# Writing the attention output of a recurrent-attention and two-layer feed-forward kernel as two column tiles of 64 tokens

## The chip, the cores and the metric

The kernel runs on one core of a Trainium2 chip. The metric is the time of the device for one execution, in microseconds (us), lower is better. Before the change it is 1050.95 us, the median of three runs (1050.66 to 1052.82).

## What is computed

For 4 batches of 8 heads, 768 tokens and a head dimension of 48, a decaying state is carried over the tokens, and its output goes through two feed-forward layers. The core of the reference is:

```python
for t in range(S):
    cur = einsum('bhd,bhe->bhde', u * k[t], v[t])
    y[t] = einsum('bhd,bhde->bhe', r[t], state + cur)
    state = w[t][..., None] * state + einsum('bhd,bhe->bhde', k[t], v[t])
x = y                    # 3072 tokens x 384
h = x @ w_in             # 384 x 2048
g = where(h >= 1, h, where(h <= -1, 0, (h + 1)**2 / 4))
x2 = g @ w_out           # 2048 x 384
out = (silu(x2 @ w_gate) * (x2 @ w_val)) @ w_out2    # 384 x 1536, 1536 x 384
```

## The kernel before, in words

The 3072 tokens are cut into 8 halves of 384 tokens (NG = 8, T = 384; two halves make one sequence), and each half into 3 windows of 128 tokens (NW = 3, WIN = 128). Inside a window the recurrence is written as matrix products: products of r and k inside the window (scores), masked, times the values, plus r times the state carried into the window.

Phase 1 runs the first feed-forward layer of half g in 16 slots (J1 = 16) and puts the attention of half g + 1 into its slots 3 to 12. In a slot TensorE (the engine that the profile calls PE) does `tile_in` (9 products on line 1039), then the slot's one or two attention pieces (`do_fill`, in the order of FILLS), then `tile_out` (9 products on line 1063). The feed-forward products are in fp32r and stream 384 columns each. The attention of half 0 has no feed-forward work to lie beside and runs at the start of the kernel. Phase 2 (from about 600 us on) runs the second feed-forward layer and has no attention in it.

The attention pieces of a window are these, with the lines of their products. All are fp32, and each product written in the code is two matmul records in the trace (a weight load and a matmul for either of two passes), except for transposes:
- KT, line 1082: k transposed, 4 transposes.
- AT, line 1089: the scores. Each of the 8 products has 48 rows of contraction, at partitions 0 to 47 for one head of a pair and 64 to 111 for the other, so the two heads lie on different halves of the array's rows. They write two banks. This is the only code of the kernel in which products occupy different parts of the array.
- ST, line 1098: the state's increment, 4 products with 112 weight columns.
- Y, lines 1104 and 1108: the output. Line 1104 multiplies r (stationary, 112 rows x 128 tokens) by the decayed state (96 columns moving), once for each of 4 pairs of heads. Line 1108 multiplies the masked scores (stationary, 128 x 128 tokens) by the values (48 columns moving), once for each of 8 heads. All write one bank: 128 tokens on the partitions, 384 columns. Where a sequence starts (window 0 of an even half) line 1104 is left out.
- XT, line 1113: the output transposed for the feed-forward layer, 3 transposes.

VectorE (DVE) drains Y on line 908 (`x_by_token`), after which XT can run one slot later. `glo` (line 916) is the product of DVE that each `tile_out` waits for.

Of the kernel before, what the change touches and what calls it, by code (L numbers as in the profile page):

```python
# [31 lines left out]
B, H, S, D = 4, 8, 768, 48  # L32
# [3 lines left out]
WIN = 128  # L36
# [47 lines left out]
def build_program(nc, w_d, kd_d, rd_d, rn_d, kn_d, vn_d, u_d, cst_d, w1i_d, w1o_d, w2g_d, w2v_d,  # L84
                  w2o_d, rs_d, ks_d, vs_d, ws_d, us_d, out_d, x2_d, ys_d):
    ctx = ExitStack()
    with ctx:
        at = [nc.sbuf_base + (-nc.sbuf_base) % 32]

        def place(name, shape, dt, offset=None):  # L90

            size = 2 if dt == mybir.dt.bfloat16 else 4
            for n in shape[1:]:
                size *= n
            if offset is None:
                offset = at[0]
                at[0] += (size + 31) // 32 * 32
            assert offset + size <= nc.sbuf_usable_end, (name, offset + size)
            return nc.alloc_sbuf_tensor_at(name, shape, dt, offset=offset), offset + size
# [32 lines left out]
        rd, _ = place("r_by_channel", [PR, NPAIR, T], F32)  # L132
# [3 lines left out]
        vn, _ = place("v_by_token", [P, NW, DM], F32)  # L136
        uu, _ = place("u_rows", [P, DM], F32)
        att = [place(f"att{i}", [P, 4, WIN], F32)[0] for i in range(2)]
        ktk = [place(f"k_token{i}", [P, NPAIR * PR], F32)[0] for i in range(2)]
        sbar, _ = place("state_decayed", [PR, NPAIR, 2 * D], F32)  # L140
# [12 lines left out]
        for n in ("hi", "lo"):  # L153
            t, o = place(f"w2gv_a{n}", [P, NA, 2, KT * P], F32R, o)
# [3 lines left out]
        for n in ("hi", "lo"):  # L158
            t, o = place(f"w2gv_b{n}", [P, J2 - NA, 2, KT * P], F32R, o)
            w2b.append(t)  # L160
        w2o = []
        for n in ("hi", "lo"):
            t, o = place(f"w2o{n}", [P, J2, DM], F32R, o)
# [55 lines left out]
        def state_pairs(w, parity):  # L219

            return 1 if parity == 1 and w == NW - 1 else NPAIR
# [26 lines left out]
        def bank_of(g, f):  # L248

            return (attb + hid + acc)[f % 8] if isinstance(g, int) and g == 0 else attb[f % NBANK]  # L250

        def cols(w):
            return slice(w * WIN, (w + 1) * WIN)
# [775 lines left out]
        @block.tensor  # L1029
        def _(e):  # L1030
            THREE = ((0, 0), (0, 1), (1, 0))

            def products(out, w_of, x_of, n, start, stop):

                total = 3 * n
                i = 0
                for k in range(n):
                    for a, b_ in THREE:
                        m = e.matmul(out, w_of(a, k), x_of(b_, k), start=start and i == 0,  # L1039
                                     stop=stop and i == total - 1)  # L1040
                        i += 1
                return m
# [10 lines left out]
            def tile_out(ph, g, j, wo):  # L1053
# [5 lines left out]
                for k in (0, 2, 1):  # L1059
                    if j == 0 and k == 1:  # L1060
                        e.wait_ge(M["ed", ph], g + 1)
                    for i, (a, b_) in enumerate(THREE):
                        m = e.matmul(acc[k][:, 0:T], wo[a][:, j, k * P:(k + 1) * P], gs[b_][:, :],  # L1063
# [3 lines left out]
            def do_fill(g, f, parity):  # L1067
                kind, w, n = FILLS[f]
                if kind == "AT" and n == 1:
                    return  # L1070
                out = bank_of(g, f)
                bank_free(g, f)
                if kind == "KT":
                    first_half = isinstance(g, int) and g == 0
                    if w == 0 and not first_half:
                        e.wait_ge(scaled, (g + 1) * (2 * NPAIR))
                    if w == 0 and isinstance(g, int) and g == 0:
                        e.wait_ge(ld["cst"], 16)
                    for p in range(NPAIR):
                        if w == 0 and first_half:  # L1080
                            e.wait_ge(scaled, 2 * p + 2)
                        m = e.transpose(out[:, p * PR:(p + 1) * PR], kd[:, p, cols(w)], ident[0:PR, 0:PR])  # L1082
                elif kind == "AT":
                    other = bank_of(g, f + 1)
                    bank_free(g, f + 1)
                    for p in range(NPAIR):
                        for i, o in enumerate((out, other)):
                            r = slice(64 * i, 64 * i + D)
                            m = e.matmul(o[:, p * WIN:(p + 1) * WIN], kd[r, p, cols(w)], rd[r, p, cols(w)],  # L1089
                                         start=True, stop=True)  # L1090
                            if p == NPAIR - 1 and i == 0:
                                m.then_inc(fill, 1)
                elif kind == "ST":
                    e.wait_ge(kt_out, g * NW + (w + 1))
                    if w == 0:
                        e.wait_ge(ld["vn"], (g + 1) * 16)
                    for p in range(state_pairs(w, parity)):
                        m = e.matmul(out[0:PR, p * 2 * D:(p + 1) * 2 * D], ktk[w % 2][:, p * PR:(p + 1) * PR],  # L1098
                                     vn[:, w, p * 2 * D:(p + 1) * 2 * D], start=True, stop=True)
                elif kind == "Y":  # L1100
                    e.wait_ge(st_dec, g * NW + (w + 1))
                    row_start = w == 0 and parity == 0
                    for p in range(0 if row_start else NPAIR):
                        e.matmul(out[:, p * 2 * D:(p + 1) * 2 * D], rd[:, p, cols(w)], sbar[:, p, :],  # L1104
                                 start=(p == 0), stop=False, skip_group_check=True)
                    e.wait_ge(at_out, g * (2 * NW) + (2 * w + 2))
                    for h in range(H):
                        m = e.matmul(out[:, h * D:(h + 1) * D], att[h % 2][:, h // 2, :], vn[:, w, h * D:(h + 1) * D],  # L1108
                                     start=(row_start and h == 0), stop=(h == H - 1), skip_group_check=True)
                elif kind == "XT":  # L1110
                    e.wait_ge(y_out, g * NW + (w + 1))
                    for k in range(KT):
                        m = e.transpose(out[:, k * P:(k + 1) * P], xn[:, w, k * P:(k + 1) * P], ident)  # L1113
                m.then_inc(fill, 1)

            def bank_free(g, f):

                n_bank = 8 if isinstance(g, int) and g == 0 else NBANK
                gg, ff = (g, f - n_bank) if f >= n_bank else (g - 1, f - n_bank + NF)
                if isinstance(gg, int) and gg < 0:  # L1120
                    return
                kind, w, n = FILLS[ff]
                if kind == "KT":
                    e.wait_ge(kt_out, gg * NW + (w + 1))
                elif kind == "AT":
                    e.wait_ge(at_out, gg * (2 * NW) + (2 * w + n + 1))
                elif kind == "ST":
                    e.wait_ge(st_out, gg * (2 * NW) + (2 * w + 2))
                elif kind == "Y":
                    e.wait_ge(y_out, gg * NW + (w + 1))  # L1130
                else:
                    e.wait_ge(xl_out, gg * NW + (w + 1))
# [3 lines left out]
            for f in range(NF):  # L1136
                do_fill(0, f, 0)
# [19 lines left out]
            def slot(g, j, parity, next_half, after_next):  # L1157
                last = isinstance(g, int) and g == NG - 1
                if j + 2 < J1:
                    tile_in(g, j + 2, parity)  # L1160
                elif not last:
                    tile_in(g + 1, j + 2 - J1, 1 - parity)
                else:
                    tile_in2(0, j + 2 - J1, 0)
                if last and j == 4:
                    e.wait_ge(w_sum, NG + 2)
                    e.matmul(attb[2][0:1, 0:1], bad[:, OPS_CHECK:OPS_CHECK + 1], ones[:, :], start=True, stop=True).then_inc(w_tot, 1)
                if next_half:
                    for f in WIN_SLOTS.get(j, ()):
                        do_fill(g + 1, f, 1 - parity)  # L1170
                tile_out(1, g, j, w1o)
# [76 lines left out]
```

## Time and profile before

| | |
|---|---|
| median of 3 runs | 1050.95 us |
| time of the profiled execution | 1050.49 us |
| its span in the trace | 1048.6 us |
| PE busy | 96% of the span |
| DVE busy | 53% |
| ACT busy | 38% |
| POOL busy | 13% |

The span is what the trace covers; the time is 1.9 us longer. An engine's row is its busy time; PE is TensorE's matmuls and PEld its weight loads, which overlap them. Since matmuls overlap each other in the records too, the cost of one is better read from the distance between starts than from its duration. PEclk is the clock granted to TensorE, in tenths of 2.4 GHz.

### The profile page before, as it was taken

The numbers are of one execution on the slowest core, as the hardware profiler recorded it, in microseconds if no ns is written. First come the engines' busy times: TensorE is split into PE (matmuls) and PEld (weight loads), VectorE is DVE, ScalarE is ACT, GpSimd is POOL, SyncE is SP. The second block draws the span as 40 slices with busy tenths as digits, with TensorE's granted clock in tenths as the row PEclk, the third lists the DMA queues.
The fourth block names the chain that finished last, engine by engine and source line by source line (L and its number), as shares of the span: only waits on it lengthen the run. The fifth ranks groups of instructions, "written<-read, shape, count | busy, mean of one in ns | idle before, by whom it ended". The sixth has DMA issues, their size and how long they took to land.

```text
span 1048.6 us, 15818 instructions
## 1 busy us (share of the span) xinstructions
PE 1004.0 (96%) x6162; PEld 990.1 (94%) x6162; DVE 555.8 (53%) x958; ACT 394.5 (38%) x799; POOL 133.6 (13%) x90
## 2 busy tenths in 40 slices
PE   1689999999999999999999999999999999999997
PEld 0679999999999999999999999999999999999997
DVE  7866584774947759477444443343434343433332
ACT  3445344453454535544366532222222222222221
POOL 4650030110301203002026320000000000000000
PEclk9989999999999999999999999999999999999999
DMA  6450140400503105030033211001010101010000
GB/s 225 149 181 27 30 142 1 144 27 3 168 1 132 39 2 170 1 121 24 1 121 98 91 53 46 2 1 46 1 45 0 45 0 45 0 45 0 23 1 25
DMA packets 23199, 59.63 MB, mean 57 GB/s; under 512 B 2657, under 2 KB 11489, under 8 KB 23137
## 3 DMA queue, kind: packets, MB, share of 16 engines
q1 hardware_dynamic: 23136, 58.79, 17.1%
q8 instruction: 41, 0.67, 0.3%
q14 instruction: 22, 0.17, 0.1%
HBM read 49.34 MB, written 9.44 MB: 56 GB/s over the span
## 4 chain that ended last, share of the span: by engine, by line
PE 92%; DVE 4%; issue 1%; ACT 1%; DMA 1%; SPq 0%; DVEq 0%; ACTq 0%
PE bank L1039 47%; PE bank L1063 34%; PE bank L1108 4%; PE bank L1089 2%; PE bank L1104 2%; PE bank L1098 1%; PE bank L1082 1%; PE bank L1113 1%; DVE w_window L835 1%; DVE r_by_channel L860 1%; DVE k_by_channel L852 1%; DVE suf L830 1%; DVE w_by_channel L843 0%; DMA w_by_channel<-in_w_channel 0%; DMA ring<-in_w_out 0%
## 5 line engine op out<-in xcount | busy, mean ns | idle before, releaser
L690 ACT ACTIVATE ghi<-gate 128x384 fp32r<-128x384 f32 x224 | 117.9, 526 | 256.7 <-PE bank L1063 111.3
L916 DVE TENSOR_TENSOR glo<-gate,ghi 128x384 fp32r<-128x384 f32 x224 | 136.5, 610 | 115.8 <-ACT ghi L690 113.4
L933 DVE TENSOR_TENSOR gate<-bank,gate 128x384 f32<-128x384 f32 x96 | 53.6, 558 | 221.6 <-ACT gate L794 221.6
L1039 PE MATMUL bank<-xlo,w2gv_ahi 128*128 128x384 f32 x480 | 162.1, 338 | 0.0
L1039 PE MATMUL bank<-xhi,w2gv_alo 128*128 128x384 f32 x480 | 162.1, 338 | 0.0
L1039 PE MATMUL bank<-xhi,w2gv_ahi 128*128 128x384 f32 x480 | 162.1, 338 | 0.0
L1063 PE MATMUL bank<-ghi,w1ohi 128*128 128x384 f32 x384 | 136.9, 357 | 3.1 <-DVE glo L916 3.1
L794 ACT ACTIVATE gate<-bank 128x384 f32<-128x384 f32 x96 | 47.3, 493 | 234.1 <-PE bank L1039 234.1
L1039 PE MATMUL bank<-xhi,w1ihi 128*128 128x384 f32 x384 | 130.7, 340 | 1.3 <-DVE xlo L911 1.3
L1039 PE MATMUL bank<-xlo,w1ihi 128*128 128x384 f32 x384 | 130.5, 340 | 0.0
L1039 PE MATMUL bank<-xhi,w1ilo 128*128 128x384 f32 x384 | 130.4, 339 | 0.0
L1063 PE MATMUL bank<-glo,w1ohi 128*128 128x384 f32 x384 | 129.7, 338 | 0.0
L1063 PE MATMUL bank<-ghi,w1olo 128*128 128x384 f32 x384 | 129.6, 338 | 0.0
L923 DVE SCALAR_TENSOR_TENSOR gate<-bank,gate 128x384 f32<-128x384 f32 x128 | 70.9, 554 | 106.5 <-ACT gate L699 106.3
L697 ACT ACTIVATE gate<-bank 128x384 f32<-128x384 f32 x128 | 62.7, 490 | 101.2 <-PE bank L1039 101.2
L1063 PE MATMUL bank<-ghi,w2ohi 128*128 128x384 f32 x288 | 97.3, 338 | 0.0
L1063 PE MATMUL bank<-ghi,w2olo 128*128 128x384 f32 x288 | 97.3, 338 | 0.0
L1063 PE MATMUL bank<-glo,w2ohi 128*128 128x384 f32 x288 | 97.3, 338 | 0.0
L1039 PEld LDWEIGHTS bank<-xhi,w2gv_alo 128*128 128x128 f32 x480 | 90.1, 188 | 0.0
L1039 PEld LDWEIGHTS bank<-xlo,w2gv_ahi 128*128 128x128 f32 x480 | 90.1, 188 | 0.0
L1039 PEld LDWEIGHTS bank<-xhi,w2gv_ahi 128*128 128x128 f32 x480 | 90.1, 188 | 0.0
L1063 PEld LDWEIGHTS bank<-ghi,w1ohi 128*128 128x128 f32 x384 | 72.2, 188 | 7.4 <-DVE glo L916 4.8
(81 smaller groups left out, 1607.9 us busy)
## 6 DMA issues: line engine op xcount, KB each, us to landing
w_by_channel<-in_w_channel SPq DMA_DIRECT2D x16, 339.5 KB, 3.8
k_by_channel<-in_k_channel SPq DMA_DIRECT2D x16, 336.0 KB, 4.8
r_by_channel<-in_r_channel SPq DMA_DIRECT2D x16, 336.0 KB, 5.5
ring<-in_w_out SPq DMA_DIRECT2D x28, 192.0 KB, 2.7
r_k_diag<-in_r_token SPq DMA_DIRECT2D x8, 576.0 KB, 7.0
k_by_token<-in_k_token SPq DMA_DIRECT2D x8, 576.0 KB, 8.0
v_by_token<-in_v_token SPq DMA_DIRECT2D x8, 576.0 KB, 9.1
x_t<-ring SPq DMA_DIRECT2D x8, 576.0 KB, 3.3
```

Source lines behind the costliest of these rows:

```text
L690: e.activation(ghi[j % 2][:, :], gate[j % 2][:, :], ACT.Copy).then_inc(M["hi", ph], 1)
L697: e.activation(q, hid[j % 2][:, 0:T], ACT.Relu, bias=0.5, scale=0.5).then_inc(M["q", 1], 1)
L794: e.activation(gate[j % 2][:, :], hid[j % 2][:, 0:T], ACT.Sigmoid).then_inc(M["q", 2], 1)
L830: e.tensor_tensor_scan(suf[:, p, ::-1], w_at[:, p, :0:-1], last_of_window[0:PR, ::-1], 0.0, ALU.mult, ALU.add).then_inc(scan, 1)
L916: e.tensor_tensor(glo[j % 2][:, :], gate[j % 2][:, :], ghi[j % 2][:, :].bitcast(F32), ALU.subtract)\
L923: e.scalar_tensor_tensor(q, hid[j % 2][:, 0:T], 1.0, q, ALU.max, ALU.min).then_inc(M["g", 1], 1)
L933: e.tensor_tensor(q, hid[j % 2][:, 0:T], q, ALU.mult).then_inc(M["t", 2], 1)
L1039: m = e.matmul(out, w_of(a, k), x_of(b_, k), start=start and i == 0, stop=stop and i == total - 1)
L1063: m = e.matmul(acc[k][:, 0:T], wo[a][:, j, k * P:(k + 1) * P], gs[b_][:, :], start=(j == 0 and i == 0), stop=(j == J[ph] - 1 and i == 2))
L1089: m = e.matmul(o[:, p * WIN:(p + 1) * WIN], kd[r, p, cols(w)], rd[r, p, cols(w)], start=True, stop=True)
L1104: e.matmul(out[:, p * 2 * D:(p + 1) * 2 * D], rd[:, p, cols(w)], sbar[:, p, :], start=(p == 0), stop=False, skip_group_check=True)
L1108: m = e.matmul(out[:, h * D:(h + 1) * D], att[h % 2][:, h // 2, :], vn[:, w, h * D:(h + 1) * D], start=(row_start and h == 0), stop=(h == ...
```

## The change

Line 1104 and line 1108 write their result in two pieces each: tokens 0 to 63 of the window to partitions 0 to 63, and tokens 64 to 127 to partitions 64 to 127. Each piece has 64 weight columns and the same moving operand as before. There are twice as many products, and the two of a pair lie on different halves of the array's columns. Bank, sums, waits and semaphores are the same; the increment that announces the fill is on the last product.

```diff
+            HALVES = (slice(0, WIN // 2), slice(WIN // 2, WIN))
...
                     for p in range(0 if row_start else NPAIR):
-                        e.matmul(out[:, p * 2 * D:(p + 1) * 2 * D], rd[:, p, cols(w)], sbar[:, p, :],
-                                 start=(p == 0), stop=False, skip_group_check=True)
+                        for t in HALVES:
+                            e.matmul(out[t, p * 2 * D:(p + 1) * 2 * D], rd[:, p, cols(w)][:, t], sbar[:, p, :],
+                                     start=(p == 0), stop=False, skip_group_check=True)
                     e.wait_ge(at_out, g * (2 * NW) + (2 * w + 2))
                     for h in range(H):
-                        m = e.matmul(out[:, h * D:(h + 1) * D], att[h % 2][:, h // 2, :], vn[:, w, h * D:(h + 1) * D],
-                                     start=(row_start and h == 0), stop=(h == H - 1), skip_group_check=True)
+                        for t in HALVES:
+                            m = e.matmul(out[t, h * D:(h + 1) * D], att[h % 2][:, h // 2, t],
+                                         vn[:, w, h * D:(h + 1) * D], start=(row_start and h == 0),
+                                         stop=(h == H - 1), skip_group_check=True)
```

## Rows read from the trace of the kernel before

**Rows 1.** The page: the span, the engines' busy time, and PE and its clock in 40 slices.
```profile
span 1048.6 us, 15818 instructions
PE 1004.0 (96%) x6162; PEld 990.1 (94%) x6162; DVE 555.8 (53%) x958; ACT 394.5 (38%) x799; POOL 133.6 (13%) x90
...
PE   1689999999999999999999999999999999999997
...
PEclk9989999999999999999999999999999999999999
```

**Rows 2.** The page: the chain that ended last, by engine and by line.
```profile
PE 92%; DVE 4%; issue 1%; ACT 1%; DMA 1%; SPq 0%; DVEq 0%; ACTq 0%
PE bank L1039 47%; PE bank L1063 34%; PE bank L1108 4%; PE bank L1089 2%; PE bank L1104 2%; PE bank L1098 1%; PE bank L1082 1%; PE bank L1113 1%; DVE w_window L835 1%; DVE r_by_channel L860 1%; DVE k_by_channel L852 1%; DVE suf L830 1%; DVE w_by_channel L843 0%; DMA w_by_channel<-in_w_channel 0%; DMA ring<-in_w_out 0%
```

**Rows 3.** Waits of PE: line, releaser, us in total, times, longest.
```profile
PE bank L1063 <- DVE glo L916: 3.1, 2, 2.9
```

**Rows 4.** PE by stretch, line 1108 alone, then line 1104 alone, from 64 us.
```profile
64.00:1049.00 985.00, 40.07 (x336) 39.20 (x336) 1.00 0.15 49
...
64.00:1049.00 985.00, 18.66 (x144) 17.92 (x144) 1.00 0.15 49
```

**Rows 5.** Timeline of PE around one Y: start, us, line, operation.
```profile
172.74 0.55 PE L1082 MATMUL bank<-cst,k_by_channel 112*128 112x112 f32 x4
173.13 1.04 PE L1104 MATMUL bank<-state_decayed,r_by_channel 112*128 112x96 f32 x8
174.01 1.91 PE L1108 MATMUL bank<-v_by_token,att 128*128 128x48 f32 x16
175.74 0.42 PE L1063 MATMUL bank<-ghi,w1ohi 128*128 128x384 f32 x1
176.00 0.34 PE L1063 MATMUL bank<-glo,w1ohi 128*128 128x384 f32 x1
```

**Rows 6.** The chain in order of time, 144 to 215 us, nine feed-forward products.
```profile
148.44 1.58 PE bank L1039 x9
```

**Rows 7.** Timeline of PE around one ST (112 weight columns).
```profile
168.79 0.93 PE L1098 MATMUL bank<-v_by_token,k_token 128*112 128x96 f32 x8
169.50 0.42 PE L1063 MATMUL bank<-ghi,w1ohi 128*128 128x384 f32 x1
169.76 0.33 PE L1063 MATMUL bank<-glo,w1ohi 128*128 128x384 f32 x1
```

**Rows 8.** Timeline of PE around one AT (products on different row halves).
```profile
163.83 0.33 PE L1039 MATMUL bank<-xhi,w1ilo 128*128 128x384 f32 x1
164.09 1.16 PE L1089 MATMUL bank<-r_by_channel,k_by_channel 48*128 48x128 f32 x16
165.19 0.44 PE L1063 MATMUL bank<-ghi,w1ohi 128*128 128x384 f32 x1
165.47 0.34 PE L1063 MATMUL bank<-glo,w1ohi 128*128 128x384 f32 x1
```

**Rows 9.** Instructions by line: shapes, count, busy us, mean ns, idle before them.
```profile
L1108 PE MATMUL bank<-v_by_token,att 128*128 128x48 f32 x384 | 49.2, 284 | 1.4 <-DVE att L894 1.4
L1082 PE MATMUL bank<-cst,k_by_channel 112*128 112x112 f32 x96 | 15.2, 277 | 23.1 <-DVE r_by_channel L860 23.1
...
L1108 PEld LDWEIGHTS bank<-v_by_token,att 128*128 128x128 f32 x384 | 48.0, 203 | 1.7 <-DVE att L894 1.7
L1082 PEld LDWEIGHTS bank<-cst,k_by_channel 112*128 112x128 f32 x96 | 12.2, 150 | 24.6 <-DVE r_by_channel L860 13.6 <-issue 10.3
```

**Rows 10.** Timeline of DVE, 166 to 194 us.
```profile
171.98 0.56 DVE L916 TENSOR_TENSOR glo<-gate,ghi 128x384 fp32r<-128x384 f32 x1 [0.57 <-ACT ghi L690]
...
175.95 0.56 DVE L908 TENSOR_TENSOR x_by_token<-bank,r_k_diag 128x384 f32<-128x384 f32 x1 [1.38 <-PE bank L1108]
```

**Rows 11.** The start: a piece of the chain, and DVE's timeline, 44 to 84 us.
```profile
48.85 3.67 PE bank L1108 x16
...
60.72 0.56 DVE L908 TENSOR_TENSOR x_by_token<-bank,r_k_diag 128x384 f32<-128x384 f32 x1
```

## The prediction

> **What bounds the kernel now.** I read the page first. TensorE is busy in nine tenths or more of every slice from the fourth to the last but one, at full clock from there on, and the other engines have room [rows 1]. The chain that ended last is PE for 92% of the span. Lines 1104 and 1108, which the change touches, are 2% and 4% of it [rows 2], so only some 60 us are at stake. Then I asked what PE waits for once it is running. Behind the feed-forward products it is two waits of 3.1 us in total [rows 3]. So a microsecond that Y gives back or takes on PE moves the end by as much, unless something else is late by then.
>
> What is the price of Y? From 64 us on there are 336 records of line 1108 and 144 of line 1104 [rows 4], in 21 Y pieces of 16 records, 18 of which have the 8 of line 1104 as well. The busy time (40.1 and 18.7 us) overstates them, since records overlap. Distances between starts are better. In one Y, line 1104 starts at 173.13, the feed-forward goes on at 175.74 and its second product starts at 176.00 [rows 5]. Nine feed-forward products take 1.58 us, 0.1756 us each [rows 6]. So 24 records took 2.87 us less one feed-forward interval, 2.69 us: **0.112 us for one record**, whether it streams 96 columns or 48 (line 1104 alone: 0.88 us for 8, 0.110). Streaming is not what it waits for, then. The weight load is, and ST shows it. Its records load 112 columns instead of 128 and stream 96; 8 of them take 169.76 - 168.79 - 0.176 = 0.794 us, 0.099 each [rows 7]. Single records 0.112 and 0.099 apart give 0.8 ns for a weight column, and for 64 columns 0.058 us (in proportion it would be 0.056).
>
> **The change, part by part.** Each record of Y becomes a pair of records on different column halves: 336 pairs on line 1108, 144 on line 1104 at full clock, and 48 and 16 in the start.
>
> (a) The pair's time. The trace of before has no two products on different column halves. It has AT, with two on different row halves: 16 records with 128 weight columns, and the feed-forward goes on 1.10 us after the first [rows 8]. At one record after another, 16 x 0.112 would be 1.79 us. So a pair on different row halves takes the place of one record: its weight loads and its streams both run side by side. That is the nearest row, and I take it for column halves as well. The other end is that the two halves run one after another, 2 x 0.058 = 0.117 us for a pair. On line 1108 a pair that runs side by side is as long as one load of 64 columns, 0.058. On line 1104 the stream shows up. Transposes (line 1082) load faster (mean 150 ns against 203) [rows 9], and 4 of them with 112 moving columns take 173.13 - 172.74 = 0.39 us, 0.097 each [rows 5]; so fp32 columns go by at about 0.86 ns, and 96 columns take 0.082 us, 48 columns 0.041. So a pair is 0.082 on line 1104, between 0.058 and 0.112. Gain: 336 x (0.112 - 0.058) = 18.0 us and 144 x (0.112 - 0.082) = 4.3 us, together **-22.3 us**.
>
> (b) The switch. Going from the whole array to a divided one and back is not free. Around AT, from the last whole-array product at 163.83 to the second one after it at 165.47 is 1.64 us [rows 8]. Take off two feed-forward intervals (0.35) and eight pairs at 0.112 (0.90), and 0.39 us is left: the first loads can't be put under the products ahead of them, on either side. Lines 1104 and 1108 stand back to back, so each Y pays once: 21 x 0.39 = **+8.2 us**. Its bounds are nothing and twice that. The Trainium skill says the same in "TensorEngine Tiling (Array Packing)", section Key Properties: changing the tiling mode drains the engine. It gives no price, and the row does.
>
> (c) The records themselves. Twice as many weight loads and matmuls have to be issued, four records for a pair in 0.058 us, 15 ns each. The nearest row is AT, four in 0.112, 28 ns each, where the load sets the pace, so it is no limit that I can read. I put it at nothing, and the case where 28 ns is the floor among the rivals.
>
> (d) What is late next. The `glo` that the feed-forward product at 175.74 needs is begun at 171.98 and done at 172.54 at the latest [rows 10], over 3 us ahead, so up to 1.3 us less on PE uncovers nothing. (The `glo` of 171.98 may even be the next slot's; then the margin is larger.) DVE's drain of Y waits 1.38 us for PE [rows 10] and comes earlier with it, and XT runs a whole slot later. The DMAs for the following half start after the last XT, so they shift along with everything. No other queue is touched.
>
> (e) The start. Y of half 0 runs partly at 1.2 GHz, and its second window is on the chain with 3.67 us [rows 11]. A gain of some 1.3 us there is followed by work of DVE, and the drain of the third window begins without any idle time ahead of it [rows 11], so DVE was late, not PE. Between 0 and -1.3 us; I take **-0.3**, near nothing, by that last row.
>
> Sum: -22.3 + 8.2 - 0.3 = **-14.4 us**. The profiled execution took 1050.49 us, 0.46 under the median, which is the same for this purpose. 1050.5 - 14.4 = **1036.1 us**, -1.4%. With no price for the switch, line 1104 at 0.058 and the whole gain in the start it is 1050.5 - 18.0 - 7.8 - 1.3 = 1023; with twice the price and line 1104 at 0.112, 1050.5 - 18.0 + 16.4 = 1049. The likeliest case's own range is 1029 to 1045.
>
> **The rivals.**
>
> A, slower: the weight loads of the two column halves follow one another. Both halves use all rows of the array, and AT's evidence is only on products that don't share rows. Then a pair costs 0.117 instead of 0.112, 480 x 0.005 = +2.4 us, and the switch comes on top: +10.6, **1061 us**. A floor of 28 ns a record gives nearly the same (+8.2, 1059). The point from which it decides: the switch costs 8.2 us over 480 pairs, 0.017 each, so the change loses as soon as a pair takes more than 0.095 us on average. For it: no row shows column halves side by side. Against it: AT's streams and loads are both doubled at no cost. The Trainium skill speaks for A in "TensorE: Matmul & The Clock Gate", section The mechanism: weight loads overlap matmuls in flight only where the row group differs. The same page tells of three column tiles that ran 2.38 times as fast, with streams of 512 columns, where loads are small; the trace shows neither.
>
> B, slower: loads side by side, but the streams one after another, as they carry the same moving data from the same partitions. A pair takes 2 x 0.041 = 0.082 on line 1108 (336 x -0.030 = -10.1) and 0.164 on line 1104 (144 x 0.052 = +7.5). With the switch it is +5.6, **1056 us**.
>
> C: the change doesn't do what it says, and the halves run as narrow products on the undivided array. There is no switch, and a pair costs 0.117: +2.4 us, **1053 us**, a hair over the bound of what can be told from no change.
>
> D: it works, but the switch is dearer than at AT, so that the two cancel (0.39 becomes 1 us): about 1050.
>
> **How the numbers follow.** Forecast 0.62; A with the floor 0.19; B 0.07; C 0.06; D 0.06. Slower by over 0.2% (A, B, and most of C) is 0.31, within 0.2% (most of D and a little of C) 0.05, faster 0.64; 0.2%, 2 us, is about what a measurement of this kernel can tell from no change. The range reaches from the forecast's low side, 1029, over D, C and B to 1057 and leaves out A and the very end of the gains, some 0.2.
>
> **What the profile of the changed kernel would show.** Right: 768 and 320 records on lines 1108 and 1104 in place of 384 and 160, starting in pairs a few ns apart; the feed-forward going on about 1.5 us after a full Y begins, not 2.6; line 1104 slower for a record than 1108; a gap of some 0.1 to 0.2 us on either side of Y as around AT. A shows in records of line 1108 evenly 0.058 apart; B in line 1104 taking twice the time of line 1108; C in the missing gaps. The sum is wrong if PE's waits at lines 1063 or 1113 grow, or if the granted clock falls in the stretches with Y, where less of the array is at work.

## The result and the profile after

The changed kernel takes 1036.4 us (median of 4, 1035.1 to 1039.6) against 1051.4 for the kernel before, a ratio of 0.986 with a 95% interval of 0.983 to 0.989: 15 us or 1.4% faster. Forecast were 1036.1 us and 14.4 us.

The page of the changed kernel, beside rows 1 and 2:

```profile
span 1033.6 us, 16906 instructions
PE 983.8 (95%) x6706; PEld 964.7 (93%) x6706; DVE 555.4 (54%) x958; ACT 394.3 (38%) x799; POOL 135.1 (13%) x90
...
PEclk9679999999999999999999999999999999999999
...
PE 91%; DVE 4%; issue 2%; DMA 1%; ACT 1%; SPq 0%; DVEq 0%; ACTq 0%
```

The bound is the same, PE for 91% of the chain. There are 544 more matmuls and as many more weight loads. In the second and third slice the row PEclk is lower than it was; the last section says why that row can't be taken at its word there.

The groups of the two lines (by line, with shapes, count, busy us and mean ns), where line 1104 has become 1106 and line 1108 has become 1111; the `128*64` is the size of the weights:

```profile
L1111 PE MATMUL bank<-v_by_token,att 128*64 128x48 f32 x768 | 27.2, 225 | 1.9 <-DVE att L894 1.9
L1106 PE MATMUL bank<-state_decayed,r_by_channel 112*64 112x96 f32 x320 | 18.8, 264 | 1.4 <-DVE state_decayed L882 1.4
```

The timeline of PE around one full Y and around one without the state's part, both at full clock; the first answers to rows 5:

```profile
105.77 0.55 PE L1083 MATMUL bank<-cst,k_by_channel 112*128 112x112 f32 x4
106.24 0.88 PE L1106 MATMUL bank<-state_decayed,r_by_channel 112*64 112x96 f32 x16
106.95 1.09 PE L1111 MATMUL bank<-v_by_token,att 128*64 128x48 f32 x32
107.97 0.44 PE L1064 MATMUL bank<-ghi,w1ohi 128*128 128x384 f32 x1
108.25 0.34 PE L1064 MATMUL bank<-glo,w1ohi 128*128 128x384 f32 x1
...
155.98 0.55 PE L1083 MATMUL bank<-cst,k_by_channel 112*128 112x112 f32 x4
156.46 1.14 PE L1111 MATMUL bank<-v_by_token,att 128*64 128x48 f32 x32
...
157.81 0.34 PE L1064 MATMUL bank<-glo,w1ohi 128*128 128x384 f32 x1
```

I read a piece from its first transpose to the second feed-forward product, since the ways in and out of the divided array lie inside these two points. Before, that was 176.00 - 172.74 = 3.26 us [rows 5]; now it is 108.25 - 105.77 = 2.48. Twice the records take 0.78 us less. Thirty-two records of line 1111 go by in 1.02 us, where 16 took 1.73.

How far does that carry? The first transposes of two later halves, in the timeline of PE after the change:

```profile
276.60 0.55 PE L1083 MATMUL bank<-cst,k_by_channel 112*128 112x112 f32 x4
...
340.94 0.55 PE L1083 MATMUL bank<-cst,k_by_channel 112*128 112x112 f32 x4
```

and the same two transposes in the kernel before:

```profile
282.95 0.55 PE L1082 MATMUL bank<-cst,k_by_channel 112*128 112x112 f32 x4
...
349.36 0.55 PE L1082 MATMUL bank<-cst,k_by_channel 112*128 112x112 f32 x4
```

A half takes 64.34 us instead of 66.41, and the following one 64.44 instead of 66.71: 2.17 us less on average, where the forecast's terms (a) and (b) make 14.1 / 7 = 2.01 for each of seven halves. PE waits for nothing in these two halves, before or after. Seven halves make 15.2 us, and the span is 15.0 us shorter. I call the time from the first transpose of one half to that of the next its period below; where nothing waits it repeats within 0.2 us from one half to the next but one, so it tells kernels apart more finely than the medians do.

### The profile page after: what moved, and what is told of

Read it like the earlier page. It is cut to its first block, busy times and chain, and to the rows that moved or that the text cites. A ratio compares the mean times of both kernels' runs of the same rounds, so it can differ in the third digit from the quotient of the medians.

```text
span 1033.6 us, 16906 instructions
## 1 busy us (share of the span) xinstructions
PE 983.8 (95%) x6706; PEld 964.7 (93%) x6706; DVE 555.4 (54%) x958; ACT 394.3 (38%) x799; POOL 135.1 (13%) x90
## 4 chain that ended last, share of the span: by engine, by line
PE 91%; DVE 4%; issue 2%; DMA 1%; ACT 1%; SPq 0%; DVEq 0%; ACTq 0%
PE bank L1040 48%; PE bank L1064 35%; PE bank L1090 2%; PE bank L1111 2%; PE bank L1106 1%; PE bank L1099 1%; PE bank L1083 1%; PE bank L1117 1%; DVE r_by_channel L860 1%; DVE k_by_channel L852 1%; DMA ring<-in_w_out 1%; DVE w_by_channel L843 1%; DVE suf L830 1%; DVE w_window L835 0%; DMA w_by_channel<-in_w_channel 0%
```

## The experiments

The theory: the two column halves of the array load and stream side by side; a pair is as long as the longer of its weight load and its stream; and each change of the array's division has a price. All times below are medians, beside the kernel before on the same chip (1050.6 to 1051.6 us); the ranges over the runs of one kernel are 1.4 to 9 us wide.

**Each part by itself.** In `e1_values_only` only the values' products are divided, in `e2_state_only` only the state's.

```diff
-                        for t in HALVES:        # line 1106 (e1) or line 1111 (e2)
+                        for t in (slice(0, WIN),):
```

> Only line 1108's part (values by scores) is divided into column halves; queries by state stays whole. Theory (pairs run side by side, 0.0584 us against 0.1117 for a whole record, and one switch of 0.32 us for each Y): 336 x 0.0533 = 17.9 us gained, 21 x 0.32 = 6.7 paid, some 1.5 gained in the start: about 1050.9 - 12.7 = 1038 us (1036 to 1041), and in the trace pairs 0.058 us apart. Rival (the gain of the change comes from something else, such as the start or the order of the feed-forward products, and the pairs save nothing): within 2 us of before.

> Only line 1104's part (queries by state) is divided; values by scores stays whole. Theory: its pairs are held by their stream of 96 columns at 0.0826 us, so 144 x 0.029 = 4.2 us gained against 18 switches of 0.32 = 5.8 paid: +1.6, about 1052 us (1050 to 1054), no gain by itself. Together with the values alone that is -9.6 away from the start, 5.8 short of the change's -15.4, which is the second switch in each of 18 pieces. Rival (each part gains by itself, and the gains simply add up to the change's 15 us): 1047 or less.

Measured: values only 1039.4 us, ratio 0.989 (0.987 to 0.991); state only 1054.0, ratio 1.002 (1.001 to 1.003). So one part carries the change and the other loses a little by itself (0.1 to 0.3%). The two pieces, values only first:

```profile
106.78 0.55 PE L1083 MATMUL bank<-cst,k_by_channel 112*128 112x112 f32 x4
107.16 1.04 PE L1106 MATMUL bank<-state_decayed,r_by_channel 112*128 112x96 f32 x8
...
109.48 0.33 PE L1064 MATMUL bank<-glo,w1ohi 128*128 128x384 f32 x1
```

and state only:

```profile
107.91 0.55 PE L1083 MATMUL bank<-cst,k_by_channel 112*128 112x112 f32 x4
108.39 0.88 PE L1106 MATMUL bank<-state_decayed,r_by_channel 112*64 112x96 f32 x16
...
111.27 0.34 PE L1064 MATMUL bank<-glo,w1ohi 128*128 128x384 f32 x1
```

From first transpose to second feed-forward product they take 2.70 and 3.36 us against 3.26 before: -0.56 and +0.10. The sum is -0.46, and both together give -0.78. The missing 0.32 us is the second switch, which the two parts share when both are divided. That is why the state's part, a loss of 0.10 alone, is worth 0.22 beside the values.

**The price of a switch by itself.** Both kernels divide the state and four heads of the values, and do four heads whole. They differ in the order alone.

```diff
# e3_four_whole: one divided stretch
-                        for t in HALVES:
+                        for t in (HALVES if h < 4 else (slice(0, WIN),)):
# e4_alternate: four divided stretches
-                        for t in HALVES:
+                        for t in (HALVES if h % 2 == 0 else (slice(0, WIN),)):
```

> Queries by state and heads 0 to 3 of the values divided, heads 4 to 7 whole: one divided stretch a Y, as in the change. Theory: 168 pairs cost 0.1117 instead of 0.0584, +9.0 us on the changed kernel: about 1045 us (1043 to 1048). Rival (the switch grows with the number of divided products): more than the 9 us is missing or given back.

> The same products, shapes and counts as the kernel with heads 4 to 7 whole, but the even heads divided and the odd heads whole, so that the array is divided and undivided four times in each Y instead of once. Theory (a switch costs 0.32 us for both ways, whatever lies between): 3 x 21 x 0.32 = +20 us on the kernel with four whole heads, about 1065 us (1060 to 1071), slower than before by 1.4%. Rival (the gap around the divided stretch comes from the feed-forward product after it and not from the switch): less than 3 us between the two.

Measured: 1043.2 us (1040.1 to 1049.0), ratio 0.993 (0.991 to 0.995), and 1060.2 us, ratio 1.009 (1.007 to 1.012). The same products cost 17.0 us more, which is 0.27 us for each of 63 ways out and in at full clock (the nine of half 0 are not counted). The timeline of PE with the four whole heads together:

```profile
105.49 0.55 PE L1083 MATMUL bank<-cst,k_by_channel 112*128 112x112 f32 x4
...
106.68 1.64 PE L1111 MATMUL bank<-v_by_token,att 128*64 128x48 f32 x24
...
108.40 0.34 PE L1064 MATMUL bank<-glo,w1ohi 128*128 128x384 f32 x1
```

and with the heads alternating:

```profile
105.19 0.55 PE L1083 MATMUL bank<-cst,k_by_channel 112*128 112x112 f32 x4
...
106.37 2.44 PE L1111 MATMUL bank<-v_by_token,att 128*64 128x48 f32 x24
...
108.89 0.34 PE L1064 MATMUL bank<-glo,w1ohi 128*128 128x384 f32 x1
```

The pieces are 2.91 and 3.70 us, 0.79 apart for three switches, 0.26 each. The way out and in costs this between short products too, so no feed-forward stream is needed to explain it, which was the rival.

The first of the two also gives a pair's time without any edge. Eight pairs became eight whole records and the piece grew from 2.48 to 2.91, 0.43 us or 0.054 each; with 0.112 for a whole record [rows 5] a pair is **0.058 us**. On the state the full piece less the piece without it is 2.48 - 1.83 = 0.65 us for 8 pairs, **0.081 us**. What is left of the piece without state, 1.83 less transposes (0.38), a feed-forward interval (0.18) and 16 pairs (0.93), is the switch between feed-forward and Y, **0.34 us**.

**Does the order of issue matter?** In `e5_half_by_half` all products of one column half come before those of the other, within each part.

```diff
-                    for p in range(0 if row_start else NPAIR):
-                        for t in HALVES:
+                    for t in HALVES:
+                        for p in range(0 if row_start else NPAIR):
...
-                    for h in range(H):
-                        for t in HALVES:
+                    for t in HALVES:
+                        for h in range(H):
```

> The same divided products as the change, but all those of tokens 0 to 63 first and then all of tokens 64 to 127 (within the state's part and within the values' part), so that neighbours in the order of issue lie on the same column half. Theory (two products run side by side only where they follow each other in the program's order, because loads and matmuls are taken up nearly in order): the pairs fall apart, a value product costs 0.058 us and a state product 0.083, 672 x 0.058 + 288 x 0.083 = 63 us against 31 in the change: about 1066 us (1060 to 1070), slower than before. This is also the price of my rival in which the halves run one after another. Rival (the two column halves have queues of their own and overlap however they are ordered): within 2 us of the change, 1037.

Beside it the changed kernel ran once more:

> The changed kernel once more, on the chip of the three that follow, as their reference: 1036 us (1034 to 1040), pairs 0.0584 us apart on the values and 0.0826 on the state.

Measured: 1036.3 us for the change again, and 1051.0 for this one, ratio to before 0.999 (0.998 to 1.001). All of the gain is gone, but not the 15 us more that full serialization would have taken, so neither theory was right as it stood. The timeline of PE shows what lies between:

```profile
104.71 1.01 PE L1106 MATMUL bank<-state_decayed,r_by_channel 112*64 112x96 f32 x13
105.48 0.26 PE L1111 MATMUL bank<-v_by_token,att 128*64 128x48 f32 x1
105.56 0.25 PE L1106 MATMUL bank<-state_decayed,r_by_channel 112*64 112x96 f32 x1
105.58 0.28 PE L1111 MATMUL bank<-v_by_token,att 128*64 128x48 f32 x2
105.64 0.25 PE L1106 MATMUL bank<-state_decayed,r_by_channel 112*64 112x96 f32 x1
...
105.73 0.25 PE L1106 MATMUL bank<-state_decayed,r_by_channel 112*64 112x96 f32 x1
105.75 1.60 PE L1111 MATMUL bank<-v_by_token,att 128*64 128x48 f32 x28
107.29 0.44 PE L1064 MATMUL bank<-ghi,w1ohi 128*128 128x384 f32 x1
```

Products of the values start at 105.48 and 105.58 while the state's last three (105.56, 105.64 and 105.73, 0.08 apart) are still to come. In the program all the state's products stand ahead. So the values' first half runs on the free column half while the state's second half is finishing, and one half does get ahead of the other, but only by some three records: where a whole group of 8 or 16 stands ahead, the rest of the other half's work waits its turn. Three more Y pieces of the trace show the same three. Y takes 2.58 us from its first record to the feed-forward, against 1.73 in the change. I didn't try how far the lead can be stretched.

**Four column tiles of 32 tokens** (`e6_quarters`):

```diff
-                        for t in HALVES:
+                        for t in QUARTERS:      # four slices of 32 tokens, in both parts
```

> Four column tiles of 32 tokens instead of two of 64, in both parts. Theory (a group of products side by side takes the longer of its load, 0.8 ns a weight column, and its stream, 0.86 ns a moving column): values 0.045 us for a group in place of 0.058, state unchanged at 0.083: 336 x 0.0135 = -4.5, about 1032 us (1030 to 1035). Rival (records can't be issued so fast: a group is 8 records, 5.6 ns each; starts within a pair are 6.7 ns apart, 4 of them 27 ns, and loads take the same again, 54): no gain on the values, and a loss if the 4 times as many records are also slow to fetch: 1036 to 1045.

Measured: 1032.3 us, ratio to before 0.981 (0.979 to 0.983), 4.1 us under the change. Its timeline:

```profile
95.33 0.55 PE L1084 MATMUL bank<-cst,k_by_channel 112*128 112x112 f32 x4
95.81 0.87 PE L1107 MATMUL bank<-state_decayed,r_by_channel 112*32 112x96 f32 x32
96.49 0.86 PE L1112 MATMUL bank<-v_by_token,att 128*32 128x48 f32 x64
...
97.57 0.34 PE L1065 MATMUL bank<-glo,w1ohi 128*128 128x384 f32 x1
```

The state's part (line 1107 there) goes from 0.71 to 0.68 us though its weights are half as wide, so it is held by its stream of 96 columns. The values' part goes from 1.02 to 0.80 for 16 groups, 0.014 a group, where 0.0135 were expected. Loads and streams thus run four abreast, and eight records can be issued in 0.05 us. (In the profiled execution the periods are 63.6 us against 64.3 to 64.4 in the change. Its start is late, which comes up again with the last kernel.)

**Sparing switches.** In `e7_beside_scores` Y stands directly ahead of AT, with the order of the pieces as it was.

```diff
+WIN_SLOTS[5], WIN_SLOTS[6] = (4,), (5, 6, 7)
+WIN_SLOTS[8], WIN_SLOTS[9] = (10,), (11, 12, 13)
```

> The change, with Y of windows 0 and 1 moved one slot later, directly ahead of AT, whose products are divided by rows; order of the pieces and all work unchanged. 14 of the 21 Y pieces at full clock then go from column halves to row halves with no feed-forward product between them. Theory (a switch is paid at each change of the array's division, about 0.16 us a way, so one of four such changes is spared): 14 x 0.16 = -2.3, about 1034 us (1032 to 1037). Rival (going from columns to rows costs as much as the two ways it replaces): the same as the change within 1 us.

Measured: 1033.6 us, ratio to before 0.983 (0.980 to 0.985), 2.7 under the change. The ranges overlap (1032.4 to 1036.9 against 1034.5 to 1036.6), so the trace has to decide:

```profile
98.65 0.34 PE L1042 MATMUL bank<-xhi,w1ilo 128*128 128x384 f32 x1
...
100.65 1.16 PE L1092 MATMUL bank<-r_by_channel,k_by_channel 48*128 48x128 f32 x16
...
102.02 0.33 PE L1066 MATMUL bank<-glo,w1ohi 128*128 128x384 f32 x1
```

From the last whole product to the second one after, Y and AT take 3.37 us together. Apart they take 1.64 for AT [rows 8] and 2.48 - 0.38 + 0.18 = 2.28 for Y (the piece above with a feed-forward product in place of the transposes), less the two feed-forward intervals (0.35) that are then counted twice: 3.57. So 0.20 us are spared, 2.8 for 14 pieces, where 2.3 were forecast: going from column halves to row halves is cheaper than going over the whole array.

Two kernels divide ST too. They compute only the diagonal blocks of the state's increment, leaving out the off-diagonal ones that nothing reads. The second also puts ST into Y's slot.

```diff
# both
-                        m = e.matmul(out[0:PR, p * 2 * D:(p + 1) * 2 * D], ktk[w % 2][:, p * PR:(p + 1) * PR],
-                                     vn[:, w, p * 2 * D:(p + 1) * 2 * D], start=True, stop=True)
+                        for i in range(2):
+                            r0, c0 = 64 * i, p * 2 * D + D * i
+                            m = e.matmul(out[r0:r0 + D, c0:c0 + D], ktk[w % 2][:, p * PR + r0:p * PR + r0 + D],
+                                         vn[:, w, c0:c0 + D], start=True, stop=True)
# e9_increment_beside: FILLS with ST 0 behind KT 1 and ST 1 behind KT 2, and
+WIN_SLOTS[4], WIN_SLOTS[5] = (2, 3), (4, 5)
+WIN_SLOTS[7], WIN_SLOTS[8] = (8, 9), (10, 11)
+WIN_SLOTS[10], WIN_SLOTS[11] = (14,), (15, 16)
```

> The change, and the state's increment (line 1098) divided as well, in its own place: of each pair of heads only the two diagonal blocks are computed (48 weight columns and 48 moving columns on either column half; the off-diagonal blocks, which nobody reads, are left out). Theory: a pair takes 0.045 us in place of 0.098 for a whole record, 144 x 0.053 = 7.6 us gained at full clock, but ST lies between whole products, so 20 more switches of 0.27 to 0.32 us, 5.4 to 6.4, are paid: -1 to -2 us on the change, about 1035 us (1033 to 1037). Rival (halving both load and stream is worth its full 8 us, since the switch is hidden under the feed-forward's long streams): 1028.

> The same products as the kernel before, but ST moved behind the next KT, so that it stands directly ahead of Y in one divided stretch. Theory: the same 7.6 us gained and no further switch: about 1036.3 - 7.6 = 1029 us (1027 to 1031), 6 less than with ST alone. Rival (the new order makes something else late, above all AT's bank or DVE's drain of the increment): PE waits at AT or Y, and 1032 or more.

> The order of the pieces of the kernel with ST beside Y (ST moved behind the next KT, into Y's slot), with ST's products whole as before: everything that the new order does, without the divided increment. Theory (the 9.7 us that the order and the divided increment brought together are the increment's 1.1 to 1.3 us a half and the switches spared, and the order itself is neutral): the same as the change, 1036 us (1034 to 1039). Rival (the order helps by itself, in the start or at the stall in the first slots of a half): 1032 or less.

Measured: alone 1036.1 us, no gain on the change; beside Y 1026.6, ratio to before 0.977 (0.976 to 0.979); the order by itself 1035.3, within the spread of the change. The three ran on two chips and the change on a third. Against the kernel before on its own chip the change is 14.8 us faster, the increment alone 14.5, the order alone 16.3 and both together 24.0. So the same products are worth nothing that shows in one place and 7.6 to 9 us in the other. The periods agree: 64.3 and 64.4 in the change in turn, 64.2 and 64.4 with the order alone, 64.0 and 64.5 with the increment alone, and 63.0 and 63.4 with both. That is 1.1 us a half and 7.6 for seven less than the order alone, the 7.6 that were expected; the order is neutral. Beside Y, ST's 16 records take 0.39 us:

```profile
105.02 0.56 PE L1104 MATMUL bank<-v_by_token,k_token 128*48 128x48 f32 x16
105.41 0.85 PE L1111 MATMUL bank<-state_decayed,r_by_channel 112*64 112x96 f32 x16
106.09 1.09 PE L1116 MATMUL bank<-v_by_token,att 128*64 128x48 f32 x32
```

That is 0.049 for a pair, against 0.099 for one whole record [rows 7].

Last, both ideas together, with ST in four tiles of 32, 16, 32 and 16 columns and Y in quarters:

> The same order, with four column tiles of 32 tokens in Y, and the increment in four tiles as well (32, 16, 32 and 16 columns), so that there is one kind of division in a stretch. Theory: the 4 us that quarters gave by themselves come on top, since only the values' groups (0.042 against 0.058) change: about 1025 us (1023 to 1027), the fastest of all. Rival (8 records for a group are issued too slowly once three kinds of products follow one another, or the smaller weight tiles let the clock fall longer in the start): 1028 or more.

Measured: **1024.9 us**, ratio to before 0.975 (0.973 to 0.977), the lowest median of all, 25.7 us under the kernel before on its chip where the change is 14.8 under. It is only 1.7 under the kernel with halves, whose range (1026.0 to 1027.4) lies within its own (1023.3 to 1027.3). In the profiled executions the quarters do give their 4 us: the seven halves together are 4.7 us shorter than with Y in halves (periods from 62.2 against from 63.0). But the first transposes of phase 1 come 4.9 us later, here first with halves and then with quarters:

```profile
82.71 0.55 PE L1086 MATMUL bank<-cst,k_by_channel 112*128 112x112 f32 x4
...
87.57 0.55 PE L1087 MATMUL bank<-cst,k_by_channel 112*128 112x112 f32 x4
```

From 60 to 88 us the granted clock is 0.85 with halves and 0.69 with quarters. The quarters need not be the reason: `e7_beside_scores`, with Y in halves, has 0.71 there and its first transposes at 86.42. In both kernels the profiled execution was the slowest of the four, so it can't say what the medians lack of the 4 us; that stays open.

## Why the prediction was right

Point by point:

- What bounds the kernel, and that a microsecond off Y is a microsecond off the end: right, behind the start. The halves are shorter by 2.17 us and the span by 15.0.
- (a) A pair runs side by side: right, and taken from AT, which is divided by rows. 0.058 on the values was forecast and 0.058 came out; on the state 0.082 and 0.081. That the first is exact is in part luck: 0.8 ns a column, taken off 0.112 for 64 columns, gives 0.061, which would have made the gain 1.0 us smaller, and in proportion it is 0.056. The reading that the state's pair is held by its stream and the values' by their load is shown by the quarters, where only the values gained.
- (b) The switch: right in kind and a little too dear. Forecast 0.39 from AT; measured 0.34 around Y, 0.32 from the two parts' sum and 0.26 to 0.27 between short products. At 0.32 the term is 6.7 us instead of 8.2. This is the term that was furthest off behind the start.
- (c) Issue costs nothing: right, with room down to eight records in 0.05 us.
- (d) Nothing is late next: right where it was argued. Behind the first slots PE waits for `glo` once, for 0.5 us (0.6 in the second execution), and for nothing else up to the end. The drain of Y, after which DVE waited 1.38 us [rows 10], waits 1.38 in the same piece of the first half of phase 1 too, and now 0.49:

```profile
108.09 0.56 DVE L908 TENSOR_TENSOR x_by_token<-bank,r_k_diag 128x384 f32<-128x384 f32 x1 [0.49 <-PE bank L1111]
```

- (e) The start: right that DVE is late there. Y is done much sooner and PE waits for the drain the longer, 3.91 us instead of 1.63 ahead of the last XT. PE's waits at that line (1113, now 1117), which were named as a sign of a wrong sum, did grow, from 7.8 to 13.5 us, all of it in the start, where they only take up what Y gave:

```profile
55.67 1.09 PE L1111 MATMUL bank<-v_by_token,att 128*64 128x48 f32 x32
60.66 0.87 PE L1117 MATMUL bank<-cst,x_by_token 128*128 128x128 f32 x3 [3.91 <-DVE x_by_token L908]
```

The size of the term can't be read. The first transposes of phase 1 start 1.7 us earlier in the profiled execution (81.17 us below) than in the one before,

```profile
82.90 0.55 PE L1082 MATMUL bank<-cst,k_by_channel 112*128 112x112 f32 x4
```

and 1.05 us earlier in the second one of the change, where -0.3 was taken. But over the 14 profiled executions they start anywhere from 80.31 to 87.57 us.

That the sum came out within 0.6 us of the measured 15.0 is therefore in part luck. Of the 15.0 us of the span, the start gave 1.4 more than forecast, and seven halves 1.1 more. Against that, the profiled execution lost two things in the first halves of phase 1 that I hadn't foreseen: 0.6 us in the half from 147 to 212 us, with the wait of 0.5 for `glo`, and 1.4 us in the first slots. There PE waits for DVE, as before, and then this time runs at the lower clock (columns: stretch, its length, busy PE, PEld, DVE, ACT, POOL, then the granted clock):

```profile
82.00:86.00 4.00, 4.00 (x26) 3.88 (x23) 4.00 (x4) 1.85 (x4) 2.37 (x1) 0.61 0.60 178
```

and the timeline of PE in the same place:

```profile
81.17 0.58 PE L1083 MATMUL bank<-cst,k_by_channel 112*128 112x112 f32 x4 [2.09 <-DVE r_by_channel L860]
...
83.16 0.52 PE L1064 MATMUL bank<-glo,w1ohi 128*128 128x384 f32 x1
83.48 0.52 PE L1064 MATMUL bank<-ghi,w1olo 128*128 128x384 f32 x1
```

After the gap of 2.09 us feed-forward products start 0.32 us apart instead of 0.18, at 1.2 GHz. About ten products at that pace cost 1.4 us. What brought the clock down is not shown: before the change PE waits 2.90 us there, in the second execution of the changed kernel 3.15, and both go on at full clock. The second execution took 1034.5 us against 1035.4.

The rivals: A and B fell with the first pairs. Even where the order of issue keeps the halves apart they overlap in part, and the kernel takes 1051 us and not A's 1061. C fell with the weights of 64 columns and the switch, D with the switch's measured price. The Trainium skill's sentence that spoke for A ("TensorE: Matmul & The Clock Gate", section The mechanism: weight loads overlap matmuls in flight only where the row group differs) isn't borne out: all column halves and quarters here share their rows, and their loads ran side by side, 0.058 us for a pair of 64-column loads. That is the time of one: in `e5_half_by_half` the 32 records of a Y without the state's part, nearly all one after another, take 1.80 us, 0.056 each.

## What to carry to other kernels

Where a small product's cost is the same whatever it streams, as here with 48 and 96 columns, look at its weight load: here it set the pace. Split the weights over column tiles, keep the tiles of a pair next to each other in the order of issue, and expect about the longer of one load and one stream, as in all the kernels here. Count the changes of division as well as the products: at about 0.3 us for the way in and out, a group of 8 pairs held by its stream lost by itself and gained beside another. So gather divided products into one stretch: here that was worth 7.6 to 9 us with the divided increment, which alone gave nothing that showed, and a finer division 4.

## What I had not expected

One column half runs ahead of the other when its neighbours in the program are all for the busy half, but only by about three records (the timeline of `e5_half_by_half`); ordering the halves one after another cost 15 us.

The row of the granted clock can't be taken at its word in the start. From 30 to 60 us it says 1.00 before the change, 0.64 in one execution of the change and 1.00 in another. But the 16 records of AT, which take 1.16 us at full clock [rows 8], take 2.08 in all three there (before the change, then its first execution; 2.08 at 50.24 us in the second), the pace of the lower clock:

```profile
52.44 2.08 PE L1089 MATMUL bank<-r_by_channel,k_by_channel 48*128 48x128 f32 x16
...
50.09 2.08 PE L1090 MATMUL bank<-r_by_channel,k_by_channel 48*128 48x128 f32 x16
```

And the AT before that takes 1.16 us in the first execution of the change (at 29.56) and 2.08 in the other two (at 32.64 and 30.64). So the row shows more of the lower clock in the very execution that ran less of the start at that clock's pace. Why is not shown. From 82 to 86 us, above, row and pace agree.

The spread of the runs (1035.1 to 1039.6 us for the change) isn't explained by the mean granted clock either: the slowest of the four has the highest, 0.990 against 0.984 to 0.986. In the profiled executions it is the start that varies, by 7 us over all kernels, while the halves behind it repeat to a few tenths.
